# Two-layer network behind attention and experts: depth of the second layer's pipeline, its first and last chunks, and who splits its weights

## The chip, the cores and the metric

The kernel runs on one core of a Trainium2 chip. The metric is the device time of one launch in microseconds (us); lower is better. TensorE is called PE in the profile, VectorE DVE, ScalarE ACT, GpSimd POOL, and SyncE SP.

## The reference

Attention with 4 sink tokens and a window of 128, then a mixture of 8 experts with one expert per token, then a two-layer network. The change touches the last stage alone:

```python
def _moe2_ref(x, w_in, w_out) -> np.ndarray:   # x (3072, 512), w_in (512, 2048), w_out (2048, 512)
    h = x @ w_in
    g = h - np.tanh(h)
    return (g @ w_out).astype(np.float32)
```

## The kernel before, in words

**Stages.** The attention runs to about 205 us of the span and scatters its token rows to their experts' regions. The experts' loop over slots of 128 tokens ends at about 556 us. What follows is the last stage, here called the second layer (functions `up2` and `down2` and their helpers).

**Split numbers.** To keep float32 accuracy, each factor is cut into a high part (a copy rounded to fp32r) and a low part (the difference), and a product is three matmuls: high with high, high with low, low with high. ScalarE makes high parts, VectorE or POOL the low ones. The weights come as quarters of 1 MB into `raw`; a quarter holds two halves of 128x1024. `split_hi` (L747) on ScalarE and `split_lo` (L1356) on POOL or the code at L1252 to L1255 on VectorE split a half. `W_IN` and `W_OUT` are the indices of w_in and w_out behind the 8 experts. `load_raw` on POOL (L1415) fetches the next quarter when both halves of the old one are split.

**Tiling.** 24 tiles of 128 tokens make 6 groups of 4. Per group the hidden width of 2048 is worked in 16 chunks of 128, so there are `STEPS` = 96 chunks in all, numbered n. For a chunk:
- PE: `up2`, 12 matmuls into one of three banks (`HB`), h for 512 tokens.
- ScalarE: `square`, then `tanh` into the one bank `MT`. VectorE: `series` (needs the square). POOL: the last step of the polynomial on `ser`, then the comparison of the square with 1/256 (`s_small`). VectorE: `curve`, three passes: the product (t), the pick of tanh or polynomial by the comparison (`COPY_PREDICATED`), and the subtraction, which gives g_raw and frees the bank. ScalarE: `g_hi`; VectorE: `g_lo`.
- PE: `down2`, for each of the 4 tiles three matmuls that add to the tile's own bank (`YB`) over the 16 chunks. Here it is called the chunk's output product.

**Order around the change.** Each engine's program is written out by hand as a loop over n. PE: `up2(n)`, in chunks 10 to 13 of a group (`TURN`) the turn of one tile of the next group's tokens (`turn_rows`), then `down2(n - 2)`. `up2(n)` waits for g_raw of chunk n - 3, `down2(m)` for g_lo of m. VectorE: `g_lo(n - 2)`, the low part of a turned tile (`tokens_lo`), in chunks 1 to 8 a half of w_out, `series(n)`, `curve(n - 1)`. Behind a group's last output product ScalarE and VectorE copy two tiles each to `raw`, and POOL stores the four by indirect DMA (`store_out`). SP loads the token rows of the next groups into `raw` behind `s_out_lo` or `s_m_turned`.

**Start.** Three tiles of group 0 are turned on PE (tile 0 was already), ScalarE copies their high parts (`tokens_hi`), VectorE makes the low parts, and the first `up2` waits for all three (L713). The gT buffers are a ring of three.

## Time and profile before

| | |
|---|---|
| median of 3 runs | 1114.25 us (1113.52 to 1114.80) |
| the profiled execution | 1115.05 us, its span 1113.3 us |
| busy: PE, DVE, ACT, POOL | 1086.2 us (98%), 606.7 (54%), 482.3 (43%), 492.8 (44%) |
| mean granted clock of TensorE | 0.992 |
| chain that ended last | PE 92%, DVE 3%, POOL 2%, ACT 1%, issue 1%, DMA 1% |
| its largest lines | L705 22%, L697 22%, L630 14%, L644 14% |

The span runs from the first to the last instruction; the execution's own time is 1.75 us longer. The shares of the busy time are means over stages; the windows and the timeline show each stage by itself. The clock is given as a share of full speed: 1 is 2.4 GHz and 0.5 is 1.2 GHz.

### The profile page before, as it was taken

Reading aid. Unit: us, or ns where it says so; the run is one execution under the profiler, and the core shown is the slowest. Engines: PE = TensorE matmul, PEld = TensorE weight load, DVE = VectorE, ACT = ScalarE, POOL = GpSimd, SP = SyncE. Lnnn points to the kernel's source line nnn. Section 1 sums busy time; section 2 is a strip of 40 time slices with the busy share of each in tenths; the row PEclk is TensorE's granted clock in tenths of the full one; section 3 lists DMA queues with packets and bytes.
Section 4 is the critical chain, followed back from the end, with each engine's and each line's share of the span. In section 5 each row is a group of like instructions: output and inputs, shape, how many; then the busy total and the mean of one; then the engine's idle time right before and its main releaser. Section 6 shows DMA issues by size and latency. Waiting matters only on the chain.

```text
span 1113.3 us, 17138 instructions
## 1 busy us (share of the span) xinstructions
PE 1086.2 (98%) x6028; PEld 878.6 (79%) x6028; DVE 606.7 (54%) x1305; ACT 482.3 (43%) x1035; POOL 492.8 (44%) x496
## 2 busy tenths in 40 slices
PE   9999997999999999999989999999999999999995
PEld 6777875888888888888867888888888888888884
DVE  6787785223322232223268666666666666666664
ACT  7898884423241424442444333333333333333332
POOL 3266534707033517481374344335335335335332
PEclk9999999999999999999999999999999999999998
DMA  8636823525124444463232110001011011001000
GB/s 282 203 120 220 255 71 143 189 67 189 47 86 160 124 133 153 136 223 123 96 96 65 29 35 14 20 20 39 10 29 38 1 39 38 1 1 39 1 1 38
DMA packets 37917, 99.44 MB, mean 89 GB/s; under 512 B 8273, under 2 KB 8401, under 8 KB 32721
## 3 DMA queue, kind: packets, MB, share of 16 engines
q1 hardware_dynamic: 29392, 52.30, 15.2%
q0 software_dynamic: 8448, 46.17, 11.9%
q8 instruction: 42, 0.69, 0.3%
q14 instruction: 35, 0.28, 0.1%
HBM read 75.84 MB, written 22.61 MB: 88 GB/s over the span
## 4 chain that ended last, share of the span: by engine, by line
PE 92%; DVE 3%; POOL 2%; ACT 1%; issue 1%; DMA 1%; POOLq 0%; SPq 0%; DVEq 0%; ACTq 0%
PE bank L705 22%; PE bank L697 22%; PE bank L630 14%; PE bank L644 14%; PE bank L446 5%; PE bank L480 4%; PE bank L462 3%; PE bank L636 2%; PE bank L617 1%; PE bank L685 1%; PE bank L524 1%; POOL sq L1452 1%; PE bank L512 1%; PE bank L504 1%; DMA sorted_x<-x_tok,dest 0%
## 5 line engine op out<-in xcount | busy, mean ns | idle before, releaser
L1359 POOL TENSOR_TENSOR weights<-raw,weights 128x1024 fp32r<-128x1024 f32 x72 | 171.3, 2400 | 201.6 <-ACT weights L753 200.5
L697 PE MATMUL bank<-mT_hi,weights 128*128 128x512 f32 x768 | 251.9, 389 | 1.7 <-DVE mT_lo L1184 1.7
L705 PE MATMUL bank<-weights,gT_hi 128*128 128x512 f32 x768 | 241.9, 396 | 6.2 <-DVE gT_lo L1241 6.0
L1451 POOL TENSOR_SCALAR ser<-ser 128x512 f32<-128x512 f32 x96 | 63.9, 665 | 286.5 <-DVE ser L1223 286.3
L705 PEld LDWEIGHTS bank<-weights,gT_hi 128*128 128x128 f32 x768 | 142.1, 189 | 40.6 <-DVE gT_lo L1241 12.2
L697 PEld LDWEIGHTS bank<-mT_hi,weights 128*128 128x128 f32 x768 | 144.2, 188 | 31.8 <-DVE mT_lo L1184 2.0
L705 PE MATMUL bank<-weights,gT_lo 128*128 128x512 f32 x384 | 150.5, 392 | 0.0
L697 PE MATMUL bank<-mT_lo,weights 128*128 128x512 f32 x384 | 149.4, 389 | 0.0
L644 PE MATMUL bank<-weights,hT_hi 128*128 128x512 f32 x464 | 148.6, 401 | 0.0
L918 ACT ACTIVATE bank<-bank 128x512 f32<-128x512 f32 x96 | 55.9, 582 | 213.5 <-DVE ser L1233 213.5
L630 PE MATMUL bank<-weights,mT_hi 128*128 128x512 f32 x464 | 147.5, 399 | 0.0
L1452 POOL TENSOR_SCALAR sq<-sq 128x512 f32<-128x512 f32 x96 | 144.6, 1506 | 0.0
L1188 DVE TENSOR_SCALAR hr<-bank 128x512 f32<-128x512 f32 x29 | 20.1, 692 | 180.3 <-PE bank L630 180.3
L1223 DVE SCALAR_TENSOR_TENSOR ser<-sq 128x512 f32<-128x512 f32 x96 | 67.0, 698 | 83.3 <-ACT sq L910 83.0
L1241 DVE TENSOR_TENSOR gT_lo<-ser,gT_hi 128x512 fp32r<-128x512 f32 x96 | 68.6, 715 | 63.6 <-ACT gT_hi L924 63.6
L761 ACT ACTIVATE prob<-prob,negmax 128x264 f32<-128x264 f32 (+1 forms) x192 | 92.9, 487 | 15.9 <-DVE negmax L975 15.8
L630 PEld LDWEIGHTS bank<-weights,mT_hi 128*128 128x128 f32 x464 | 84.9, 189 | 15.9
L910 ACT ACTIVATE sq<-bank 128x512 f32<-128x512 f32 x96 | 57.3, 597 | 90.2 <-PE bank L697 90.1
L644 PEld LDWEIGHTS bank<-weights,hT_hi 128*128 128x128 f32 x464 | 82.8, 189 | 14.1
L630 PE MATMUL bank<-weights,mT_lo 128*128 128x512 f32 x232 | 91.0, 392 | 0.0
L644 PE MATMUL bank<-weights,hT_lo 128*128 128x512 f32 x232 | 90.8, 391 | 0.0
L705 PEld LDWEIGHTS bank<-weights,gT_lo 128*128 128x128 f32 x384 | 72.4, 189 | 15.7
(154 smaller groups left out, 1584.4 us busy)
## 6 DMA issues: line engine op xcount, KB each, us to landing
raw<-w_all POOLq DMA_DIRECT2D x32, 1024.0 KB, 5.5
raw<-w_all SPq DMA_DIRECT2D x8, 1024.0 KB, 7.6
sorted_y<-ys SPq DMA_DIRECT2D x30, 257.0 KB, 3.3
xs<-sorted_x SPq DMA_DIRECT2D x29, 257.0 KB, 2.8
kT<-kt SPq DMA_DIRECT2D x24, 264.0 KB, 3.1
qT<-qt SPq DMA_DIRECT2D x24, 256.0 KB, 3.9
v_in<-vt SPq DMA_DIRECT2D x24, 256.0 KB, 4.0
raw<-sorted_y SPq DMA_DIRECT2D x20, 257.0 KB, 2.7
```

The lines of the kernel that those rows point to most:

```text
L630: done = e.matmul(bank[MH[n]][:, :], xp[:, c, :], wt[:, c, n * 512:(n + 1) * 512], start=(c == 0 and m == 0), stop=(c == CH - 1 and m == 2))
L644: done = e.matmul(bank[MY][:, :], xp[:, c, :], wt[:, c, :], start=(c == 0 and m == 0), stop=(c == FCH - 1 and m == 2))
L697: done = e.matmul(bank[HB[n % 3]][:, :], wt[:, f // 2, c, cols], x[:, c, :], start=(c == 0 and m == 0), stop=(c == CH - 1 and m == 2))
L705: done = e.matmul(bank[YB[i]][:, :], x[:, n % 3, rows], wt[:, f, :], start=(f == 0 and m == 0), stop=(f == GCH - 1 and m == 2))
L761: e.activation(row, row, ACT.Exp, bias=negmax[:, g % 2, h:h + 1], scale=-1.0, accum_out=rowsum[:, g % 2, h:h + 1]).then_inc(s_exp, 1)
L910: e.activation(sq[:, n % 2, :], bank[HB[n % 3]][:, :], ACT.Square).then_inc(s_sq, 1)
L918: e.activation(bank[MT][:, :], bank[HB[n % 3]][:, :], ACT.Tanh).then_inc(s_tanh, 1)
L1223: e.scalar_tensor_tensor(out=ser[:, n % 2, :], in0=sq[:, n % 2, :], scalar=SERIES_1 / SERIES_2, in1=sq[:, n % 2, :], op0=ALU.add, op1=ALU. ...
L1241: e.tensor_tensor(gT_lo[:, n % 3, :], ser[:, n % 2, :], gT_hi[:, n % 3, :].bitcast(F32), ALU.subtract).then_inc(s_glo, 1)
L1359: e.tensor_tensor(lo, src, hi.bitcast(F32), ALU.subtract).then_inc(s_w_lo, 1)
L1451: e.tensor_scalar(row, row, SERIES_2, 1.0, ALU.mult, ALU.add).then_inc(s_ser, 1)
L1452: e.tensor_scalar(u, u, SMALL_U, None, ALU.is_gt).then_inc(s_small, 1)
```

## The change

- **Depth.** Output products run three chunks behind (`DEPTH`) in place of two. The last two chunks' output products are put tile by tile: both for tile 0, then both for tile 1, and so on.
- **First chunk.** `up2` takes its eight matmuls with high parts of the tokens first and the four with low parts last, in every chunk. The first one waits for the three high parts, of which VectorE copies tile 2's, and before its ninth matmul for the low parts.
- **Comparison.** For chunks 0 and 95 VectorE makes the comparison in place of POOL.
- **Weights.** POOL splits low halves 0 to 4 of w_in and 0 of w_out, all before chunk 0; VectorE halves 5 to 7 of w_in (behind chunks 2, 4, 6) and 1 to 7 of w_out (behind 3, 5, 7 to 11). Before, POOL did all of w_in (the last two at chunks 1 and 2), and VectorE all of w_out. ScalarE's high halves of w_out follow the list `HI_AT`, and POOL's last two loads stand at chunks 3 and 7.
- **VectorE's order.** Up to chunk 11 `g_lo` stands at the end of its own step; in the last two steps the passes of chunks 94 and 95 are interleaved.
- Copies and stores of a group move one step later in each loop; those of the last group stand behind it.

`curve` is cut into `curve_t`, `curve_pick` and `curve_g`, its three passes; `w_in_lo(y)` and `w_out_lo(y)` split half y; `y_copy` is the old copy of a tile under a name.

```diff
-    STEPS, TURN = GROUPS * GCH, 10
+    STEPS, TURN, DEPTH = GROUPS * GCH, 10, 3
+    IN_POOL = 5
...
                     if j == 1:
-                        e.wait_ge(s_out_lo, 2 * i + 2)
+                        if i == 0:
+                            e.wait_ge(s_w_lo, 8 * W_IN + IN_POOL + 1)
+                        e.wait_ge(s_out_lo, 2 * i + 1)
                     else:
...
-                for c in range(CH):
-                    for m, (wt, x) in enumerate(((wih, mT_hi[j % 2]), (wih, mT_lo[j % 2]), (wil, mT_hi[j % 2]))):
-                        done = e.matmul(bank[HB[n % 3]][:, :], wt[:, f // 2, c, cols], x[:, c, :],
-                                        start=(c == 0 and m == 0), stop=(c == CH - 1 and m == 2))
+                high = [(wt, mT_hi[j % 2], c) for c in range(CH) for wt in (wih, wil)]
+                low = [(wih, mT_lo[j % 2], c) for c in range(CH)]
+                for m, (wt, x, c) in enumerate(high + low):
+                    if n == 0 and m == len(high):
+                        e.wait_ge(s_m_lo, GROUP - 1)
+                    done = e.matmul(bank[HB[n % 3]][:, :], wt[:, f // 2, c, cols], x[:, c, :],
+                                    start=(m == 0), stop=(m == 3 * CH - 1))
                 done.then_inc(s_up, 1)
...
-            e.wait_ge(s_m_lo, GROUP - 1)
-            for n in range(STEPS + 2):
+            e.wait_ge(s_m_hi, 2)
+            e.wait_ge(s_m_hi_dve, 1)
+            for n in range(STEPS + DEPTH - 2):
...
                 if n < STEPS:
                     if j == 0 and f % 2 == 0:
-                        e.wait_ge(s_w_lo, 8 * W_IN + f // 2 + 1)
+                        if f // 2 < IN_POOL:
+                            e.wait_ge(s_w_lo, 8 * W_IN + f // 2 + 1)
+                        else:
+                            e.wait_ge(s_in_lo, f // 2 - IN_POOL + 1)
                     if f == 0 and j:
...
+                if n >= DEPTH:
+                    m = n - DEPTH
                     e.wait_ge(s_glo, m + 1)
-                    if m < GCH and m % 2 == 0:
-                        e.wait_ge(s_out_lo, m // 2 + 1)
+                    if m == 0:
+                        e.wait_ge(s_w_lo, 8 * W_IN + IN_POOL + 1)
+                    elif m < GCH and m % 2 == 0:
+                        e.wait_ge(s_out_lo, m // 2)
...
+            e.wait_ge(s_glo, STEPS - 1)
+            for i in range(GROUP):
+                down2(STEPS - 2, i)
+                e.wait_ge(s_glo, STEPS)
+                down2(STEPS - 1, i)
...
+            HI_AT = (1, 3, 5, 7, 8, 9, 10)
...
-            for i, bk in ((1, MT), (2, HB[2]), (3, HB[1])):
+            for i, bk in ((1, MT), (3, HB[1])):
                 tokens_hi(0, i, bk)
             e.wait_ge(s_expert, E)
             split_hi(W_OUT, 0)
...
-                if 1 <= n < 8:
-                    split_hi(W_OUT, n)
+                if n in HI_AT:
+                    split_hi(W_OUT, 1 + HI_AT.index(n))
+                if n < STEPS:
+                    square(n)
+                    tanh(n)
                 if n == 1:
                     e.wait_ge(s_row_ids, GROUP)
                     e.wait_ge(y_all, 1)
-                    g_hi(0)
-                    square(1)
-                    tanh(1)
-                else:
-                    if n < STEPS:
-                        square(n)
-                        tanh(n)
-                    if 2 <= n <= STEPS:
-                        g_hi(n - 1)
...
+                if 1 <= n <= STEPS:
...
+            y_copy(GROUPS - 1, 1, GROUP * (STEPS - 2) + 4)
+            y_copy(GROUPS - 1, 3, GROUP * STEPS)
...
-                e.wait_ge(s_m_hi, GROUP * j + i)
+                if j:
+                    e.wait_ge(s_m_hi, GROUP * j + i - 1)
+                elif i == 2:
+                    e.wait_ge(s_m_hi_dve, 1)
+                else:
+                    e.wait_ge(s_m_hi, (i + 1) // 2)
...
+            def small(n):
+                e.wait_ge(s_w, n + 1)
+                u = sq[:, n % 2, :]
+                e.tensor_scalar(u, u, SMALL_U, None, ALU.is_gt).then_inc(s_small_dve, 1)
...
-                e.wait_ge(s_small, n + 1)
+                if n in (0, STEPS - 1):
+                    e.wait_ge(s_small_dve, 1 if n == 0 else 2)
+                else:
+                    e.wait_ge(s_small, n)
                 e.copy_predicated(row, sq[:, n % 2, :].bitcast(I32), bank[MT][:, :]).then_inc(s_cp, 1)
...
+            e.wait_ge(s_m_turned, 2)
+            e.tensor_copy(mT_hi[0][:, :, 2 * P:3 * P], by_chunk(HB[2])).then_inc(s_m_hi_dve, 1)
             for i, bk in ((1, MT), (2, HB[2]), (3, HB[1])):
                 tokens_lo(0, i, bk)
...
-                if 3 <= n:
+                if 13 <= n < STEPS or n == STEPS + 1:
                     g_lo(n - 2)
...
-                if 1 <= n <= 8:
-                    src, hi, lo = w_half(W_OUT, n - 1)
-                    e.wait_ge(s_w_hi, 8 * W_OUT + n)
-                    e.tensor_tensor(lo, src, hi.bitcast(F32), ALU.subtract).then_inc(s_out_lo, 1)
-                if n == 1:
+                if n == 0:
+                    series(0)
+                    small(0)
+                elif n == 1:
                     curve(0)
+                    series(1)
                     g_lo(0)
-                    series(1)
-                else:
-                    if n < STEPS:
-                        series(n)
-                    if 2 <= n <= STEPS:
-                        curve(n - 1)
-                if n >= 2 and (n - 2) % GCH == GCH - 1:
-                    j2 = (n - 2) // GCH
+                elif n < STEPS - 1:
+                    series(n)
+                    curve(n - 1)
+                    if n in (2, 4, 6):
+                        w_in_lo(IN_POOL + n // 2 - 1)
+                    elif n in (3, 5):
+                        w_out_lo((n - 1) // 2)
+                    elif n <= 11:
+                        w_out_lo(n - 4)
+                    if n <= 11:
+                        g_lo(n - 1)
+                elif n == STEPS - 1:
+                    curve_t(n - 1)
+                    curve_pick(n - 1)
+                    series(n)
+                    curve_g(n - 1)
+                    small(n)
+                elif n == STEPS:
+                    curve_t(n - 1)
+                    g_lo(n - 2)
+                    curve_pick(n - 1)
+                    curve_g(n - 1)
+                if n >= DEPTH and (n - DEPTH) % GCH == GCH - 1:
...
                 nxt = x + 1
-                for j in range(4 if nxt < W_IN else 3):
+                for j in range(4 if nxt < W_IN else 2):
                     split_lo(nxt, 2 * j)
                     split_lo(nxt, 2 * j + 1)
                     e.wait_ge(s_w_lo, 8 * nxt + 2 * j + 2)
                     load_raw(nxt + 1, j)
+            split_lo(W_IN, 4)
+            split_lo(W_OUT, 0)
...
-                    e.tensor_scalar(u, u, SMALL_U, None, ALU.is_gt).then_inc(s_small, 1)
-                if n == 1:
-                    split_lo(W_IN, 6)
-                if n == 2:
-                    split_lo(W_IN, 7)
-                    e.wait_ge(s_w_lo, 8 * W_IN + 8)
+                    if 0 < n < STEPS - 1:
+                        e.tensor_scalar(u, u, SMALL_U, None, ALU.is_gt).then_inc(s_small, 1)
+                if n == 3:
+                    e.wait_ge(s_w_lo, 8 * W_IN + IN_POOL)
+                    e.wait_ge(s_in_lo, 1)
+                    load_raw(W_OUT, 2)
+                if n == 7:
+                    e.wait_ge(s_in_lo, 3)
                     load_raw(W_OUT, 3)
                 if n < STEPS and j + 1 < GROUPS and TURN <= f < TURN + GROUP:
                     e.wait_ge(rows_in[f - TURN], 16 * (j + 1))
                     keep_ids(j + 1, f - TURN)
...
-                if n >= 2 and (n - 2) % GCH == GCH - 1:
+                if n >= DEPTH and (n - DEPTH) % GCH == GCH - 1:
                     for i in range(GROUP):
-                        store_out((n - 2) // GCH, i)
+                        store_out((n - DEPTH) // GCH, i)
+            for i in range(GROUP):
+                store_out(GROUPS - 1, i)
```

The order on PE from the third chunk's end to the fourth's product, before (names: `weights0` holds w_in, `weights1` w_out; banks 1 to 3 are `HB`, 4 to 7 `YB`):

```order
L697 MATMUL bank3<-mT_lo0,weights0 128x512
L697 MATMUL bank3<-mT_hi0,weights0 128x512
L705 MATMUL bank4<-weights1,gT_hi 128x512 [waits w_out_lo,g_lo]
L705 MATMUL bank4<-weights1,gT_hi 128x512
L705 MATMUL bank4<-weights1,gT_lo 128x512
L705 MATMUL bank5<-weights1,gT_hi 128x512 x2
L705 MATMUL bank5<-weights1,gT_lo 128x512
L705 MATMUL bank6<-weights1,gT_hi 128x512 x2
L705 MATMUL bank6<-weights1,gT_lo 128x512
L705 MATMUL bank7<-weights1,gT_hi 128x512 x2
L705 MATMUL bank7<-weights1,gT_lo 128x512
L697 MATMUL bank1<-mT_hi0,weights0 128x512 [waits g_raw]
```

and in the changed kernel, from the first chunk's low parts on:

```order
L707 MATMUL bank1<-mT_lo0,weights0 128x512 [waits m_lo]
L707 MATMUL bank1<-mT_lo0,weights0 128x512 x3
L707 MATMUL bank2<-mT_hi0,weights0 128x512 x8
L707 MATMUL bank2<-mT_lo0,weights0 128x512 x4
L707 MATMUL bank3<-mT_hi0,weights0 128x512 [waits w_lo]
L707 MATMUL bank3<-mT_hi0,weights0 128x512 x7
L707 MATMUL bank3<-mT_lo0,weights0 128x512 x4
L707 MATMUL bank1<-mT_hi0,weights0 128x512 [waits g_raw]
L707 MATMUL bank1<-mT_hi0,weights0 128x512 x7
L707 MATMUL bank1<-mT_lo0,weights0 128x512 x4
L715 MATMUL bank4<-weights1,gT_hi 128x512 [waits w_lo,g_lo]
L715 MATMUL bank4<-weights1,gT_hi 128x512
```

The fourth chunk's product (bank 1, behind `g_raw`) stands ahead of the first output product (bank 4, behind `g_lo`), and the first chunk waits for low parts only at its ninth matmul.

The order on VectorE at the end of the program, before (bank 2 is chunk 94, bank 3 chunk 95, bank 0 `MT`, banks 4 and 6 the output of tiles 0 and 2):

```order
L1223 SCALAR_TENSOR_TENSOR ser<-sq 128x512 [waits g_lo,sq]
L1230 TENSOR_TENSOR ser<-bank2,ser 128x512 [waits tanh,series]
L1233 COPY_PREDICATED ser<-sq,bank0 128x512 [waits small,t]
L1235 TENSOR_TENSOR ser<-bank2,ser 128x512 [waits t_picked]
L1241 TENSOR_TENSOR gT_lo<-ser,gT_hi 128x512 [waits down,g_hi]
L1230 TENSOR_TENSOR ser<-bank3,ser 128x512 [waits tanh,series]
L1233 COPY_PREDICATED ser<-sq,bank0 128x512 [waits small,t]
L1235 TENSOR_TENSOR ser<-bank3,ser 128x512 [waits t_picked]
L1241 TENSOR_TENSOR gT_lo<-ser,gT_hi 128x512 [waits down,g_hi]
L1273 COPY raw<-bank4 128x512 [waits out_done0,down]
L1273 COPY raw<-bank6 128x512 [waits out_done2,down]
```

and in the changed kernel:

```order
L1278 TENSOR_TENSOR ser<-bank2,ser 128x512 [waits tanh,series]
L1287 COPY_PREDICATED ser<-sq,bank0 128x512 [waits small,t]
L1256 SCALAR_TENSOR_TENSOR ser<-sq 128x512 [waits g_lo,sq]
L1292 TENSOR_TENSOR ser<-bank2,ser 128x512 [waits t_picked]
L1262 TENSOR_SCALAR sq<-sq 128x512 [waits series_w]
L1278 TENSOR_TENSOR ser<-bank3,ser 128x512 [waits tanh,series]
L1311 TENSOR_TENSOR gT_lo<-ser,gT_hi 128x512 [waits down,g_hi]
L1287 COPY_PREDICATED ser<-sq,bank0 128x512 [waits small_by_vector,t]
L1292 TENSOR_TENSOR ser<-bank3,ser 128x512 [waits t_picked]
L1311 TENSOR_TENSOR gT_lo<-ser,gT_hi 128x512 [waits down,g_hi]
L1300 COPY raw<-bank4 128x512 [waits down,out_done0]
L1300 COPY raw<-bank6 128x512 [waits down,out_done2]
```

The product and pick of chunk 94 went ahead of chunk 95's series, the comparison of chunk 95 (`TENSOR_SCALAR`) came in, and chunk 95's product stands ahead of chunk 94's low part.

## Rows read from the trace of the kernel before

**Rows 1.** stretches: us, busy (x count) of PE, PEld, DVE, ACT, POOL; clock; DMA share; GB/s
```profile
560.00:600.00 40.00, 36.72 (x151) 29.14 (x152) 29.58 (x36) 17.05 (x26) 26.50 (x23) 0.96 0.28 93
600.00:1089.00 489.00, 488.81 (x2184) 401.49 (x2183) 322.03 (x470) 173.98 (x294) 206.95 (x215) 1.00 0.07 21
```

**Rows 2.** timeline of PE, second layer's start: start us, us, engine line op [idle before <-releaser]
```profile
556.65 1.53 PE L685 MATMUL bank<-ident,rows 128*128 128x128 f32 x12
559.91 0.50 PE L697 MATMUL bank<-mT_hi,weights 128*128 128x512 f32 x1 [1.74 <-DVE mT_lo L1184]
...
567.98 0.39 PE L697 MATMUL bank<-mT_hi,weights 128*128 128x512 f32 x1
570.51 0.90 PE L705 MATMUL bank<-weights,gT_hi 128*128 128x512 f32 x2 [2.14 <-DVE gT_lo L1241]
...
574.94 0.40 PE L697 MATMUL bank<-mT_hi,weights 128*128 128x512 f32 x1
```

**Rows 3.** timeline of ACT, DVE and POOL, from 557 to 569 us
```profile
557.04 4.71 POOL L1359 TENSOR_TENSOR weights<-raw,weights 128x1024 fp32r<-128x1024 f32 x2
...
557.98 1.89 DVE L1184 TENSOR_TENSOR mT_lo<-bank,mT_hi 128x512 fp32r<-128x512 f32 x3 [4.81 <-ACT mT_hi L904]
...
562.97 0.60 ACT L910 ACTIVATE sq<-bank 128x512 f32<-128x512 f32 x1 [3.10 <-PE bank L697]
...
564.21 1.22 DVE L1255 TENSOR_TENSOR weights<-raw,weights 128x1024 fp32r<-128x1024 f32 x1
...
567.51 0.75 DVE L1233 COPY_PREDICATED ser<-sq,bank 128x512 f32<-128x512 int32 x1 [0.88 <-POOL sq L1452]
568.29 0.69 DVE L1235 TENSOR_TENSOR ser<-bank,ser 128x512 f32<-128x512 f32 x1
...
564.38 1.52 POOL L1451 TENSOR_SCALAR ser<-ser 128x512 f32<-128x512 f32 x1 [1.24 <-DVE ser L1223]
```

**Rows 4.** timeline of PE, two later waits of that start
```profile
583.68 0.72 PE L705 MATMUL bank<-weights,gT_hi 128*128 128x512 f32 x2 [0.36 <-DVE gT_lo L1241]
...
590.22 0.73 PE L705 MATMUL bank<-weights,gT_hi 128*128 128x512 f32 x2 [0.79 <-DVE gT_lo L1241]
```

**Rows 5.** timeline of PE, after the last of a group's four turns
```profile
730.53 0.39 PE L697 MATMUL bank<-mT_hi,weights 128*128 128x512 f32 x1
730.96 0.74 PE L705 MATMUL bank<-weights,gT_hi 128*128 128x512 f32 x2
...
752.94 0.74 PE L705 MATMUL bank<-weights,gT_hi 128*128 128x512 f32 x2
```

**Rows 6.** timeline of PE, end of the second layer
```profile
1095.02 0.39 PE L705 MATMUL bank<-weights,gT_lo 128*128 128x512 f32 x1
1097.60 0.73 PE L705 MATMUL bank<-weights,gT_hi 128*128 128x512 f32 x2 [2.19 <-DVE gT_lo L1241]
...
1101.10 0.73 PE L705 MATMUL bank<-weights,gT_hi 128*128 128x512 f32 x2 [0.48 <-DVE gT_lo L1241]
...
1103.75 0.39 PE L705 MATMUL bank<-weights,gT_lo 128*128 128x512 f32 x1
```

**Rows 7.** timeline of DVE and POOL, end of the second layer
```profile
1091.42 0.69 DVE L1241 TENSOR_TENSOR gT_lo<-ser,gT_hi 128x512 fp32r<-128x512 f32 x1 [0.70 <-ACT gT_hi L924]
...
1094.13 0.62 POOL L1451 TENSOR_SCALAR ser<-ser 128x512 f32<-128x512 f32 x1 [3.36 <-DVE ser L1223]
```

**Rows 8.** timeline of DVE, ACT and POOL, the last group's copies and stores
```profile
1102.10 0.69 DVE L1273 COPY raw<-bank 128x512 f32<-128x512 f32 x1 [1.06 <-PE bank L705]
...
1104.17 0.60 ACT L956 ACTIVATE raw<-bank 128x512 f32<-128x512 f32 x1 [0.78 <-PE bank L705]
...
1103.58 1.06 POOL L1439 DMA_INDIRECT out<-raw,ids  x1 [7.37 <-ACT raw L956]
...
1107.48 0.96 POOL L1439 DMA_INDIRECT out<-raw,ids  x1 [0.30 <-issue]
```

**Rows 9.** timeline of DVE, a half of w_out while POOL made a comparison
```profile
583.54 2.51 DVE L1255 TENSOR_TENSOR weights<-raw,weights 128x1024 fp32r<-128x1024 f32 x1
```

57 lines of the change are left out of this document (40 added, 17 removed).

## The prediction

> **What bounds the kernel now.** I read first the stretches of the span, then TensorE's timeline where it is not full, then the engines it waits for. From 600 to 1089 us PE is busy 488.81 of 489.00 us at full clock [rows 1]: nothing there can be gained except by fewer or shorter matmuls, and the change makes neither. From 560 to 600 us it is busy 36.72 of 40 us, with a mean granted clock of 0.96 [rows 1]. So the change can act at four places only: the start of the second layer, tiny lags at each group of tokens, its end, and the tail behind the last matmul. A chunk's product is 12 matmuls; their starts stand 0.23 us apart, and 2.72 us is 12 of them.
>
> The start, in PE's rows [rows 2]: the turns run from 556.65 for 1.53 us, then PE sits idle 1.74 us until VectorE's third low part of the tokens, and begins chunk 0 at 559.91. The third chunk's last matmul starts at 567.98. The first output product starts at 570.51, after 2.14 us idle, waiting for gT_lo of chunk 0; it is not over until 574.94, though 12 matmuls should take 2.72. Its two matmuls at 570.51 take 0.90 us, two plain ones 0.39 + 0.23 = 0.62: the half clock, 1.2 in place of 2.4 GHz. Two more idle pieces follow, of 0.36 and 0.79 us [rows 4].
>
> Why gT_lo of chunk 0 is late [rows 3]: ScalarE squares at 562.97, VectorE's series ends by 564.3, POOL's step on `ser` takes 1.52 us from 564.38, then POOL makes the comparison, and the pick at 567.51 has waited 0.88 us for it; g_raw is there at 568.29 + 0.69 = 568.98; ScalarE's g_hi and VectorE's g_lo follow, and PE goes on at 570.51.
>
> The end [rows 6, 7]: the chain from chunk 95's product to its g_lo is serial, and PE idles 2.19 and 0.48 us before the last two output products. Then [rows 8] tile 3 is copied at 1104.17 to 1104.77, but its store starts at 1107.48: POOL issues the four stores (1107.48 - 1103.58) / 3 = 1.30 us apart, while tiles come 0.68 apart.
>
> **The change part by part.** An idle piece costs PE its idle time and some more: 1095.02 to 1097.60 is 2.58 us, less 0.23 is 2.35, against 2.19 idle (0.16 more), and the first two matmuls behind it take 0.73 in place of 0.62 (0.12 with rounding) [rows 6].
>
> *1. Chunk 0 starts on high parts.* ScalarE copies tiles 1 and 3, VectorE tile 2 beside it, and PE waits for these three alone. The turns end at 556.65 + 1.53 = 558.18; tile 3's copy of 0.60 us (the plain ScalarE copy of a bank [rows 8]) ends at about 558.8, so chunk 0 starts at 558.85. VectorE makes tile 2's copy (0.69, as its other passes over a bank [rows 3]) by 558.4, since the second turn of the three ends at about 557.7, then three low parts, which took 1.89 together [rows 3]: done by 560.3. PE's eight high parts run to 558.85 + 8 x 0.23 = 560.7, so the low parts are in time. **Gain 559.91 - 558.85 = 1.06 us.** That the same 12 matmuls stand in another order costs nothing: each has its own weight load either way.
>
> *2. Three chunks deep.* PE now puts chunk 3's product where the first output product stood. It needs g_raw of chunk 0 alone, which frees bank 1. Everything moves 1.06 earlier: square from 561.91 to 562.51, series to 563.23, POOL's step 0.62 (its plain duration [rows 7]) to 563.93; VectorE makes the comparison itself meanwhile (0.69 or less). Then three passes, 0.69 + 0.75 + 0.69 with 0.02 between [rows 3]: g_raw at 566.15. Chunk 3 is due after 36 matmuls and the first one's 0.11: 558.85 + 8.16 + 0.11 = 567.12. It is early by 1 us. The low half of w_out that VectorE made at 564.21 (1.22 us [rows 3]) is no longer in this chain: POOL makes it ahead. Its two halves of w_in from 557.04 took 4.71 us [rows 3], 2.36 each; now the first is w_in's, to 559.4, the second w_out's, behind ScalarE's high half (ready near 559.9), to 562.3. Then it copies four ids and is free for 563.3. The first output product is due at 569.8 and its g_lo is ready near 567.5. So 567.98 + 0.23 = 568.21 to 574.94, 6.73 us, becomes 2.72. **Gain 4.0 us**, of which 2.3 is the wait and 1.7 the half clock behind it. I take it that the clock stays: what is left of idle is 558.18 to 558.85.
>
> *3. The halves of chunks 2 to 11.* VectorE takes ten halves (three of w_in, seven of w_out) in place of eight, POOL two fewer. They stand behind the three passes of the curve, where VectorE otherwise idled 0.7 us for ScalarE's g_hi. A step of VectorE is then 4 x 0.69 + 0.75 + 1.22 = 4.73 us of work [rows 3] against PE's 5.44 (two products), so it keeps up, and each g_lo has 2.72 us more than before. The two waits at 583.68 and 590.22 go: 0.36 + 0.79 + 2 x (0.16 + 0.12) = 1.71. **Gain 1.7 us.** In chunks 10 and 11 the halves now meet the turns of the next group: from the durations I find the low part of a turned tile ready 2.2 us after the chunk's product ends, due after 0.44 (the turn) + 2.72 = 3.16. POOL's two weight loads move from the expert stage and chunk 2 to chunks 3 and 7, and their high halves are not asked for before chunks 7 and 9, over 10 us later. SP's first row loads wait for the halves of their quarter, the last one for chunk 11's; its tile is turned after chunk 13. Nothing else is queued behind these. Cost 0.
>
> *4. Each later group.* Once per group, after the last turned tile, the output product starts 0.20 late (730.53 to 730.96 is 0.43, not 0.23) and its first matmuls cost 0.12 more; the first product of the next group again 0.12 (0.74 at 752.94) [rows 5]. Both wait for g_lo, and now g_lo has a product's time more. Five groups x 0.44: **gain 2.2 us.** The stores and copies of a group keep their place behind the same product.
>
> *5. The end.* Let T be the end of chunk 95's product: one output product before 1095.02 + 0.23, so 1092.53. Before, three output products follow it, now four, two whole and two by tiles; the total is the same, so only idle time counts. The new order on VectorE, with the passes' durations: g_lo of 93 at T - 1.1 [rows 7]; t and pick of 94 to T + 0.9; series 95 to T + 1.6; g of 94, then the comparison, to T + 2.6 or 2.8; POOL's step on `ser` lies beside them (0.62 [rows 7]). Then t of 95, g_lo of 94, pick and g of 95 to T + 5.4; g_hi (0.6) and g_lo: T + 6.8. PE wants it after 2 products and one tile, T + 6.12. It idles 0.7, with 0.12 behind it 0.8, where it lost 2.19 + 0.48 + 2 x (0.16 + 0.12) = 3.23. **Gain 2.4 us.**
>
> *6. The tail.* The tiles now come 1.36 us apart, slower than POOL's 1.30 per store, so the last store follows its own copy. The first store of the group started at 1103.58, 0.8 us after the first copy's end at 1102.10 + 0.69; with that delay store 3 starts 0.8 behind copy 3, where it was 1107.48 - 1104.77 = 2.71 [rows 8]. **Gain 1.9 us** (2.5 if the delay is 0.2, as from tile 1's copy, which ends 0.6 behind tile 0's).
>
> Sum: 1.06 + 4.0 + 1.7 + 2.2 + 2.4 + 1.9 = 13.3 us. The profiled execution took 1115.05, 0.8 above the median of 1114.25. 1115.05 - 13.3 = 1101.8, and 1101.0 from the median; I take **1101.3 us**.
>
> Two costs no row shows. The comparison on VectorE with operands in SBUF: above, a pass of 0.69; the lower end is 0, and either fits. And whether it disturbs POOL's step on `ser`, which runs beside it. POOL's step took 1.52 at 564.38, beside VectorE's half at 564.21 [rows 3], and 0.62 at 1094.13 [rows 7]: so between 0 and 0.9 at each of the two places. In the start 0.9 eats the 1 us in hand; at the end it puts up to 0.7 on the last g_lo. I take 0, since at the end POOL starts while VectorE is still in its pass on a bank, as in the row of 0.62.
>
> The Trainium skill (SBUF — State Buffer, on the shared port pair) says the two engines lock each other out for whole instructions when VectorE uses both ports or reads two SBUF operands. The 1.52 here and the half of 2.51 us at 583.54 against 1.22 [rows 3, 9] agree: that half ran beside a comparison on POOL. By it the comparison holds POOL off at the start, but there the time in hand covers it.
>
> **Rivals.**
> *A, the clock falls all the same.* PE still stands idle near 558.5, behind turns. For: the only fall in this layer, 0.96 of 40 us being some 3.4 us at half speed, came behind idle time [rows 1, 2]. Against: the larger idle of 1.74 brought none until the second one. Price 1.7: 1103.0. The skill (TensorE: Matmul & The Clock Gate) adds that transposes do not count as busy, which would make 556.65 to 558.85 one empty piece; in this trace 556.65 to 559.91 was longer and the clock held.
> *B, VectorE and POOL in each other's way.* If halves take 2.51 [rows 9], a step of VectorE is 4.73 + 1.29 = 6.0 against 5.44; ten steps lose 5.8, less 2.7 of slack: 3. With 0.7 at the end: 1105.0.
> *C, the wait only changes its place.* If g_raw of chunk 0 comes 2 us or more later than I find, PE idles before chunk 3 and the clock falls as before; 4.0 are not gained: 1105.3.
> *D, slower.* POOL's stores of a group hold it for four times 1.3 us [rows 8], and the next chunk's step on `ser` stands behind them. If the deeper order let that reach PE, before a product that waits for g_raw, each of five groups could stall. It decides only beyond 13.3 / 5 = 2.7 us per group; at 4 us it ends at 1121. Against: stores, copies and product keep their relative order.
> That the change does not do what it says: the order of instructions shows that it does.
>
> **Numbers.** Forecast 0.68 (including its ends of 1099.6 and 1102.3), A 0.11, B 0.09, C 0.08, D 0.02, others 0.02. The range of 8 in 10 goes from 1099.5, with the tail's 2.5 and an end without idle, to 1105.0, taking in A, the bounds and B's own value. Measurement tells 0.2%, 2.2 us, from nothing; all but D lie beyond it: faster 0.96, same 0.02, slower 0.02.
>
> **What would show it.** Chunk 0's product starts about 1.1 us earlier behind the turns; no idle PE before chunk 3; clock 1.00 from 560 to 600; no wait for gT_lo before the last tile pieces, and one of 0.5 to 1 there; the last store some 0.8 behind its copy. A wait at chunk 3, a second wait in the last tiles, or halves of 2 us and more would make it wrong.

## The result and the profile after

The changed kernel takes 1100.39 us (median of 4 runs, 1099.89 to 1101.56), the kernel before 1114.53 us beside it: ratio 0.9874, 95% interval 0.9858 to 0.9889, so 14 us (1.3%) faster. The forecast was 1101.3 us, with a range of 1099.5 to 1105.0. The profiled execution has a span of 1098.7 us.

The stretches of the changed kernel's span, with the columns of [rows 1]:

```profile
560.00:600.00 40.00, 40.00 (x178) 33.12 (x177) 34.30 (x47) 18.83 (x30) 20.92 (x24) 1.00 0.22 79
600.00:1080.00 480.00, 480.00 (x2157) 397.48 (x2156) 321.11 (x468) 173.48 (x293) 207.01 (x213) 1.00 0.07 22
```

From 560 to 600 us PE is full at a clock of 1.00, where it was busy 36.72 us at 0.96 [rows 1]; from 600 to 1080 it is busy without a gap. Its only idle pieces left in the second layer are these two (timeline of PE, start us, us, engine, line, operation, idle before and releaser):

```profile
556.31 1.53 PE L691 MATMUL bank<-ident,rows 128*128 128x128 f32 x12
558.53 2.12 PE L707 MATMUL bank<-mT_hi,weights 128*128 128x512 f32 x8 [0.69 <-ACT mT_hi L926]
560.48 1.07 PE L707 MATMUL bank<-mT_lo,weights 128*128 128x512 f32 x4
...
566.83 1.98 PE L707 MATMUL bank<-mT_hi,weights 128*128 128x512 f32 x8
...
569.55 0.62 PE L715 MATMUL bank<-weights,gT_hi 128*128 128x512 f32 x2
...
1085.51 0.39 PE L715 MATMUL bank<-weights,gT_lo 128*128 128x512 f32 x1
1086.16 0.74 PE L715 MATMUL bank<-weights,gT_hi 128*128 128x512 f32 x2 [0.27 <-DVE gT_lo L1311]
```

They answer to [rows 2] and [rows 6]. Chunk 0 starts 2.22 us after the first turn (before 3.26). Its low parts at 560.48 do not wait. Chunk 3's product begins at 566.83, right behind chunk 2's, and the first output product at 569.55, both without a bracket, so without idle time. At the end 0.27 us are left of 2.19 and 0.48, ahead of the last chunk's product with tile 0.

What releases chunk 3's product, in the timelines of DVE and POOL, against [rows 3]:

```profile
562.22 0.71 DVE L1256 SCALAR_TENSOR_TENSOR ser<-sq 128x512 f32<-128x512 f32 x1 [2.29 <-ACT sq L932]
562.96 0.43 DVE L1262 TENSOR_SCALAR sq<-sq 128x512 f32<-128x512 f32 x1
563.90 0.69 DVE L1278 TENSOR_TENSOR ser<-bank,ser 128x512 f32<-128x512 f32 x1 [0.52 <-POOL ser L1538]
564.63 0.74 DVE L1287 COPY_PREDICATED ser<-sq,bank 128x512 f32<-128x512 int32 x1
565.41 0.69 DVE L1292 TENSOR_TENSOR ser<-bank,ser 128x512 f32<-128x512 f32 x1
...
563.02 0.85 POOL L1538 TENSOR_SCALAR ser<-ser 128x512 f32<-128x512 f32 x1 [0.64 <-DVE ser L1256]
```

VectorE's comparison (L1262) takes 0.43 us and lies beside POOL's step on `ser`, which takes 0.85. The pick at 564.63 waits for nothing, and g_raw is ready at 566.10.

The tail, against [rows 8], timelines of ACT and POOL:

```profile
1091.31 0.60 ACT L948 ACTIVATE raw<-bank 128x512 f32<-128x512 f32 x1 [2.12 <-PE bank L715]
...
1088.70 1.06 POOL L1526 DMA_INDIRECT out<-raw,ids  x1 [6.85 <-DVE raw L1300]
...
1092.81 0.96 POOL L1526 DMA_INDIRECT out<-raw,ids  x1 [0.30 <-issue]
```

The last store starts 0.90 us behind the copy of tile 3 (1091.91); before it was 2.71.

**Where the 14.6 us of span went.** The stretches are measured between the same events in both traces. One output product lasts 2.72 us; the changed kernel carries one more of them from the second stretch to the fourth, and the table corrects for it:

| stretch | before | after | gain | forecast |
|---|---|---|---|---|
| first turn to chunk 0 | 3.26 | 2.22 | 1.04 | 1.06 |
| chunk 0 to the output product behind the first turn of the next group, the carried one added | 58.00 | 49.46 + 2.72 | 5.82 | 5.7 |
| from there to the end of chunk 95's product | 474.62 | 471.62 | 3.00 | 2.2 |
| from there to the last matmul, the carried output product taken off | 11.22 | 11.22 - 2.72 | 2.72 | 2.4 |
| last matmul to the last store | 3.73 | 1.98 | 1.75 | 1.9 |

Together the gains are 14.3 us. Another 0.34 lie ahead of the first turn, where the two programs are alike but for POOL's halves.

### The profile page after: what moved, and what is told of

Same layout as the page of the kernel before. It is cut to its first block, busy times and chain, and to the rows that moved or that the text cites. A ratio compares the mean times of both kernels' runs of the same rounds, so it can differ in the third digit from the quotient of the medians.

```text
span 1098.7 us, 17140 instructions
## 1 busy us (share of the span) xinstructions
PE 1079.1 (98%) x6028; PEld 877.5 (80%) x6028; DVE 609.1 (55%) x1310; ACT 481.7 (44%) x1034; POOL 484.0 (44%) x492
## 4 chain that ended last, share of the span: by engine, by line
PE 95%; DVE 1%; DMA 1%; issue 1%; ACT 1%; SPq 0%; POOL 0%; POOLq 0%; ACTq 0%; DVEq 0%
PE bank L707 24%; PE bank L715 23%; PE bank L636 15%; PE bank L650 15%; PE bank L452 5%; PE bank L486 4%; PE bank L468 3%; PE bank L642 2%; PE bank L623 1%; PE bank L691 1%; PE bank L530 1%; PE bank L518 1%; PE bank L510 1%; DMA qT<-qt 0%; DMA sorted_x<-x_tok,dest 0%
## 5 line engine op out<-in xcount | busy, mean ns | idle before, releaser
L1444 POOL TENSOR_TENSOR weights<-raw,weights 128x1024 fp32r<-128x1024 f32 x70 | 166.6, 2401 | 201.7 <-ACT weights L775 200.6
L715 PE MATMUL bank<-weights,gT_hi 128*128 128x512 f32 x768 | 238.6, 392 | 0.3 <-DVE gT_lo L1311 0.3
L707 PE MATMUL bank<-mT_hi,weights 128*128 128x512 f32 x768 | 189.8, 389 | 0.7 <-ACT mT_hi L926 0.7
L1540 POOL TENSOR_SCALAR sq<-sq 128x512 f32<-128x512 f32 x94 | 140.6, 1496 | 0.0
L707 PE MATMUL bank<-mT_lo,weights 128*128 128x512 f32 x384 | 102.7, 389 | 0.0
L650 PEld LDWEIGHTS bank<-weights,hT_hi 128*128 128x128 f32 x464 | 82.9, 189 | 14.1
```

Of the source, the lines that this page charges most:

```text
L650: done = e.matmul(bank[MY][:, :], xp[:, c, :], wt[:, c, :], start=(c == 0 and m == 0), stop=(c == FCH - 1 and m == 2))
L707: done = e.matmul(bank[HB[n % 3]][:, :], wt[:, f // 2, c, cols], x[:, c, :], start=(m == 0), stop=(m == 3 * CH - 1))
L715: done = e.matmul(bank[YB[i]][:, :], x[:, n % 3, rows], wt[:, f, :], start=(f == 0 and m == 0), stop=(f == GCH - 1 and m == 2))
L1444: e.tensor_tensor(lo, src, hi.bitcast(F32), ALU.subtract).then_inc(s_w_lo, 1)
L1540: e.tensor_scalar(u, u, SMALL_U, None, ALU.is_gt).then_inc(s_small, 1)
```

## The experiments

The part of the program ahead of the second layer ends at another time in each execution (the first turn starts between 554.9 and 558.9 us, and the clock falls once, twice or not at all in the attention). So beside the timing I compare one length within the profile: **L, from the start of chunk 0's product to the start of the last matmul**. It is 543.84 us before, 532.30 after, and 532.28 in the changed kernel's second profile (e12), so in these two it repeats to 0.02 us. L leaves out the wait ahead of chunk 0 and the stores at the end. Each value of L comes from one profiled execution.

### The end by tiles undone (e1)

```diff
             e.wait_ge(s_glo, STEPS - 1)
-            for i in range(GROUP):
-                down2(STEPS - 2, i)
-                e.wait_ge(s_glo, STEPS)
-                down2(STEPS - 1, i)
+            for n in (STEPS - 2, STEPS - 1):
+                e.wait_ge(s_glo, n + 1)
+                for i in range(GROUP):
+                    down2(n, i)
...
```

The waits of the last four copies are fitted to this order.

> The changed kernel with the last two output products whole again (chunk 94 for all four tiles, then chunk 95), nothing else. My theory: PE loses its last idle piece (0.27 us in the changed kernel's trace, 0.55 with what lies around it), since three whole products last 8.2 us and chunk 95's low part is there after 6.5; but the tiles come 0.68 us apart again, POOL's stores 1.3, so the last store starts 2.7 us behind the copy of tile 3 instead of 0.9. Sum 1.8 - 0.55 = 1.3 us slower, about 1101.6. Rival: the order by tiles is there against PE's wait and the stores do not matter; then it is as fast or 0.5 us faster, and the last store starts 0.9 us behind its copy.

Measured: 1099.92 us, ratio 0.9878 (0.9862 to 0.9895). L is 531.76, 0.54 shorter, and PE has no idle piece at the end. The stores (timelines of ACT and POOL):

```profile
1089.68 0.60 ACT L947 ACTIVATE raw<-bank 128x512 f32<-128x512 f32 x1 [0.76 <-PE bank L715]
...
1089.12 1.06 POOL L1525 DMA_INDIRECT out<-raw,ids  x1 [8.35 <-ACT raw L947]
...
1093.01 0.96 POOL L1525 DMA_INDIRECT out<-raw,ids  x1 [0.30 <-issue]
```

The last store starts 2.73 us behind the last copy (1090.28). So both halves of the theory hold in the profile: 1.83 us are lost at the stores and 0.54 won on PE, 1.3 us in sum. The timing cannot tell 1.3 us from nothing: its interval holds the changed kernel's ratio. In the profile the order by tiles pays through the stores, not through PE's wait.

### Depth two (e2) and depth alone (e8)

e2 is the changed kernel with

```diff
-    STEPS, TURN, DEPTH = GROUPS * GCH, 10, 3
+    STEPS, TURN, DEPTH = GROUPS * GCH, 10, 2
```

and the loops of copies and stores bounded to fit; e8 is the kernel before, its 2 replaced by such a `DEPTH` of 3 in PE's loop and in the copies and stores, and nothing else.

> The changed kernel with depth 2 instead of 3, all else kept (first chunk, split of the halves, VectorE's order, order by tiles at the end). My theory: PE idles about 1.2 us before the first output product (its low part was ready at 567.94, chunk 2's product ends at 566.7), 0.3 around it; the lags once or twice per group return, 2.5 us; at the end 2.7 us return. Sum 7.0 us, 1107.4, with the clock at 1.00 from 560 to 600 us; if an idle piece of 1.2 us is enough to bring the clock down, 1.7 more, 1109.1. Rival: the moved halves and VectorE's order made the gain and depth little: then within 2 us of the changed kernel.

> The kernel before with depth 3 alone: no high parts first, no halves moved, VectorE's and ScalarE's orders as before, last products whole. My theory: depth is the largest part. Chunk 3's product waits for g_raw of chunk 0, 568.98 against 568.21, so PE idles 0.6 us (0.3 more around it) where it lost 4.0; the two later waits (1.7) and the lags of the groups (2.4) go; at the end about 0.3 us idle are left of 3.2 lost. Gain 3.1 + 1.7 + 2.4 + 2.6 = 9.8 us, about 1104.3. Rival: without the new order VectorE and POOL stay late in the first chunks, PE waits for g_raw instead of g_lo at several of chunks 3 to 8, and the gain is 6 us or less, 1108.

Measured, e2: 1109.60 us, ratio 0.9961 (0.9947 to 0.9975), L 542.20, so 9.9 us of 11.5 are gone. PE's waits in its timeline:

```profile
567.42 0.73 PE L715 MATMUL bank<-weights,gT_hi 128*128 128x512 f32 x2 [0.98 <-DVE gT_lo L1311]
...
618.82 0.73 PE L715 MATMUL bank<-weights,gT_hi 128*128 128x512 f32 x2 [0.76 <-DVE gT_lo L1311]
...
1091.11 0.74 PE L715 MATMUL bank<-weights,gT_hi 128*128 128x512 f32 x2 [0.89 <-DVE gT_lo L1311]
...
1093.87 0.73 PE L715 MATMUL bank<-weights,gT_hi 128*128 128x512 f32 x2 [1.80 <-DVE gT_lo L1311]
```

The first wait is 0.98, near the 1.2 expected, and the clock holds behind it. I had not expected the 0.76 us behind the second turn (chunk 11), where a half of w_out stands ahead of g_lo on VectorE, nor the fall of the clock at 1094.9 for 3.4 us, behind the two idle pieces at the end. They make most of the difference between 9.9 and 7.0.

Measured, e8: 1110.57 us, ratio 0.9938 (0.9921 to 0.9954), on a chip where the kernel before takes 1117.97. L is 537.31: 6.5 us won, not 9.8. **The rival's mechanism is the one that came**, with a gain a little above its 6. PE now waits for g_raw, four times in the first chunks:

```profile
570.59 0.50 PE L697 MATMUL bank<-mT_hi,weights 128*128 128x512 f32 x1 [0.65 <-DVE ser L1235]
...
577.82 0.47 PE L697 MATMUL bank<-mT_hi,weights 128*128 128x512 f32 x1 [1.49 <-DVE ser L1235]
...
583.79 0.50 PE L697 MATMUL bank<-mT_hi,weights 128*128 128x512 f32 x1 [0.25 <-DVE ser L1235]
...
590.40 0.47 PE L697 MATMUL bank<-mT_hi,weights 128*128 128x512 f32 x1 [0.86 <-DVE ser L1235]
```

and once more, 0.40 us, at the first turn of the next group. The chain of that stretch (what each piece of work waited for, followed back from the end) runs from ScalarE's g_hi of chunk 0 over VectorE's g_lo of chunk 0 and its series of chunk 1 to POOL, and stays on POOL until its load at 584.61 (start us, us, what):

```profile
570.65 0.64 ACT gT_hi L924
...
571.32 0.69 DVE gT_lo L1241
572.01 0.61 DVE ser L1223
...
572.69 1.53 POOL ser L1451
574.22 1.89 POOL sq L1452
576.11 2.33 POOL weights L1359
578.44 1.09 POOL ser L1451
579.53 2.42 POOL sq L1452
581.96 2.37 POOL weights L1359
```

The step on `ser` takes 1.53 and 1.09 us for 0.62, the comparison 1.89 and 2.42 for 1.49, and between them stand w_in's halves of 2.33 and 2.37. So depth alone brings 6.5 of 11.5 us of L, all the rest without it 1.6, and 3.4 come only when both are there. By the stretches of the table in the section on the result, with gains against the kernel before:

| stretch | changed kernel | depth two (e2) | depth alone (e8) |
|---|---|---|---|
| chunk 0 to the output product behind the first turn | 5.82 | 4.08 | 0.80 |
| from there to the end of chunk 95's product | 3.00 | -0.83 | 2.98 |
| from there to the last matmul | 2.72 | -1.61 | 2.75 |

The gains at the groups and at the end come with depth alone in full. At the start it is the other way round: most of the gain is there without the third chunk of depth, and depth alone brings little.

The first of e8's four waits can be accounted for. g_raw of chunk 0 is ready 9.05 us after chunk 0's start, in the changed kernel 7.57. The comparison on POOL makes 0.59 of the difference (e4, below), and POOL's step, 1.52 us beside VectorE's half of w_out in place of the 0.62 of e4, makes the other 0.90.

### Which of the rest (e9, e10)

e9: POOL makes halves 6 and 7 of w_in at chunks 1 and 2 again. e10: VectorE's old order in chunks 2 to 11.

```diff
...
-                    if n in (2, 4, 6):
-                        w_in_lo(IN_POOL + n // 2 - 1)
+                    if n == 2:
+                        w_in_lo(IN_POOL)
+                    elif n in (4, 6):
+                        pass
...
+                if n in (1, 2):
+                    split_lo(W_IN, 5 + n)
...
```

```diff
-                if 13 <= n < STEPS or n == STEPS + 1:
+                if 3 <= n < STEPS or n == STEPS + 1:
                     g_lo(n - 2)
...
-                    series(n)
-                    curve(n - 1)
                     if n in (2, 4, 6):
                         w_in_lo(IN_POOL + n // 2 - 1)
                     elif n in (3, 5):
                         w_out_lo((n - 1) // 2)
                     elif n <= 11:
                         w_out_lo(n - 4)
-                    if n <= 11:
-                        g_lo(n - 1)
+                    series(n)
+                    curve(n - 1)
```

> The changed kernel, but POOL splits halves 6 and 7 of w_in again, at chunks 1 and 2, as in the kernel before; all else kept. It asks what made depth alone (e8) wait for g_raw. Theory P: POOL's two halves, 2.4 us each, stand ahead of its step on ser for chunks 2 and 3 and make g_raw late; then PE waits before chunks 4 to 6, some 2 us or more in sum. Theory V: it is VectorE's half standing ahead of series, beside POOL's work. By the durations in the changed kernel's trace, POOL's step of chunk 2 would come at 571.7 and of chunk 3 at 576.2, both before VectorE asks for them at 573.8 and 578.4: then PE does not wait, 0 to 0.3 us slower.

> The changed kernel, but in chunks 2 to 11 VectorE's order is the old one: g_lo of two chunks back first, then the half of the weights, then series, then the curve. POOL has no halves there. Theory V: the half delays series, POOL's step and comparison run beside the next half, both are drawn out (2.5 us instead of 1.22 for a half), and PE waits before several chunks for g_raw: 2 us or more slower. Theory P: POOL's halves were the cause in e8; then here PE has no wait in chunks 3 to 12, 0 to 0.3 us slower.

Measured, e9: 1099.21 us, ratio 0.9871 (0.9855 to 0.9888), L 532.35: nothing is lost, though the two engines do stretch each other (timelines of POOL and DVE):

```profile
567.86 2.40 POOL L1446 TENSOR_TENSOR weights<-raw,weights 128x1024 fp32r<-128x1024 f32 x1
570.23 1.59 POOL L1540 TENSOR_SCALAR ser<-ser 128x512 f32<-128x512 f32 x1
571.79 1.93 POOL L1542 TENSOR_SCALAR sq<-sq 128x512 f32<-128x512 f32 x1
...
569.56 1.78 DVE L1267 TENSOR_TENSOR weights<-raw,weights 128x1024 fp32r<-128x1024 f32 x1
571.27 1.10 DVE L1311 TENSOR_TENSOR gT_lo<-ser,gT_hi 128x512 fp32r<-128x512 f32 x1
```

POOL's step is 1.59, VectorE's half 1.78.

Measured, e10: 1100.57 us, ratio 0.9883 (0.9867 to 0.99), L 533.51, 1.2 longer, all in one wait at the first turn:

```profile
609.33 0.66 PE L691 MATMUL bank<-ident,raw 128*128 128x128 f32 x4 [0.94 <-DVE ser L1292]
```

So neither P nor V, put back by itself, brings e8's waits. In the changed kernel each delay fits into what is in hand: POOL's halves wholly, VectorE's order except at the first turn.

Beside the new chunk 0, both runs keep one thing that e8 lacks, and no run tests it alone: the order at chunk 1. In e8, as in the kernel before, ScalarE makes g_hi of chunk 0 ahead of chunk 1's square, and VectorE g_lo of chunk 0 ahead of chunk 1's series. So chunk 1's square starts 9.70 us after chunk 0's start in e8 (571.19) and 5.78 after it in the changed kernel (564.31). POOL's step for chunk 1 starts 11.20 us after it in e8, and 8.25, 8.25 and 8.24 in the changed kernel, e9 and e10. POOL's and VectorE's halves thus meet 3 us more in hand in e9 and e10 than in e8; 1.48 of them are chunk 0's earlier g_raw, the rest goes with that order. Which combination of this order, the halves, and POOL's comparison and the half at chunk 0 makes e8's later waits was not tried and stays open.

### The start: waiting for the low parts (e3)

```diff
+                if n == 0:
+                    e.wait_ge(s_m_lo, GROUP - 1)
                 for m, (wt, x, c) in enumerate(high + low):
-                    if n == 0 and m == len(high):
-                        e.wait_ge(s_m_lo, GROUP - 1)
```

> The changed kernel, but chunk 0 waits for the three low parts before its first matmul; the order of the matmuls and VectorE's copy of tile 2 stay. My theory: chunk 0 starts when the third low part ends, 559.93 in the changed kernel's trace, so at 559.97 instead of 558.53: 1.4 us slower, 1101.8, and nothing else moves, since everything behind shifts with it. Rival: the longer idle piece behind the turns brings the clock down soon after: 1.7 more, 1103.5.

Measured: 1101.59 us, ratio 0.9898 (0.9882 to 0.9915). Chunk 0 starts 3.76 us after the first turn, 1.54 later; L is unchanged at 532.28. Timeline of PE, and the stretch behind it:

```profile
559.78 2.06 PE L706 MATMUL bank<-mT_hi,weights 128*128 128x512 f32 x8 [2.23 <-DVE mT_lo L1211]
560.00:600.00 40.00, 40.00 (x178) 33.10 (x178) 33.19 (x45) 18.58 (x29) 19.37 (x23) 1.00 0.19 65
```

The idle piece of 2.23 us behind the turns brings no fall. Expected was a start 1.4 us later and no fall.

### The comparison back on POOL (e4)

In the edit, `small(0)` and `small(95)` leave VectorE and POOL makes all 96 comparisons.

> The changed kernel with the comparisons of chunks 0 and 95 on POOL again. My theory: the comparison on VectorE is worth almost nothing, since three chunks of depth leave g_raw of chunk 0 early enough: POOL's step (0.62 alone) and comparison (1.49) end at about 565.1, the pick starts 0.5 us later, g_raw is ready at 566.6 and due at 566.75. At the end POOL's comparison would be ready at 1083.3, where the pick started at 1083.25. So 0 to 0.2 us slower, 1100.5. Rival: POOL's comparison is drawn out beside VectorE (1.93 us at 567.37) or counts in full: PE idles 0.4 us or more before chunk 3, and at the end 0.5 more: 1101.3 or above.

Measured: 1100.24 us, ratio 0.988 (0.9863 to 0.9896), L 532.59, 0.29 longer. Timelines of DVE and POOL:

```profile
566.28 0.74 DVE L1284 COPY_PREDICATED ser<-sq,bank 128x512 f32<-128x512 int32 x1 [0.88 <-POOL sq L1535]
567.05 0.69 DVE L1289 TENSOR_TENSOR ser<-bank,ser 128x512 f32<-128x512 f32 x1
...
564.06 0.62 POOL L1533 TENSOR_SCALAR ser<-ser 128x512 f32<-128x512 f32 x1 [0.64 <-DVE ser L1256]
564.66 1.52 POOL L1535 TENSOR_SCALAR sq<-sq 128x512 f32<-128x512 f32 x1
```

The pick waits 0.88 us for POOL as before the change, g_raw comes 0.59 later against chunk 0's start (8.16 for 7.57), and PE still does not wait before chunk 3; at the end its idle piece is 0.44 instead of 0.27. So the comparison on VectorE is worth 0.3 us of L, too little for the timing. POOL's step takes 0.62 here, 0.85 with the comparison on VectorE beside it: that 0.23 is the cost that I had bounded by 0 and 0.9 and taken as 0.

### What an idle piece costs (e5, e6, e7)

One more wait ahead of chunk 3's product in the changed kernel, on `s_glo, 1`, on `s_w, 3` and on `s_graw, 2`:

```diff
                     if n >= 3:
                         e.wait_ge(s_graw, n - 2)
+                    if n == 3:
+                        e.wait_ge(s_glo, 1)
```

> The changed kernel with one added wait: chunk 3's product also waits for the low part of chunk 0 (there at 567.94; chunk 2's product ends at 566.7). It prices a short idle piece of PE. My theory: PE idles 1.2 us, 0.3 more around it, the clock stays at 1.00 behind it: 1.5 us slower, 1101.9. Rival: the idle piece is enough for a fall of the clock: 1.7 more, 1103.6.

> The changed kernel with one added wait: chunk 3's product also waits for VectorE's series of chunk 2 (there at 568.95). PE idles 2.2 us, as long as before the first output product of the old kernel. My theory, by the old kernel's trace, where 2.14 us idle were followed by a fall: the clock falls to half for 3.4 us, 2.2 + 0.3 + 1.7 = 4.2 us slower, 1104.6. Rival: it was the two idle pieces within 10 us of each other, 1.74 and 2.14, that brought it down, and here with 0.69 and 2.2 it stays: 2.5 us slower, 1102.9.

> The changed kernel with one added wait: chunk 3's product also waits for g_raw of chunk 1 (there at 571.06). PE idles 4.3 us. My theory: the clock falls for 3.4 us, once: 4.3 + 0.3 + 1.7 = 6.3 us slower, 1106.7. Rival: the fall lies within the idle piece itself and costs nothing beyond it, 4.6 us slower, 1105.0.

Measured: 1104.06, 1107.03 and 1109.96 us, ratios 0.988 (0.9863 to 0.9896), 0.9905 (0.9888 to 0.9922) and 0.9927 (0.991 to 0.9944), on the chip of e8. L is 533.66, 536.28 and 539.59. Timelines of PE, for e6 with one window behind the wait, for e7 with three, one across the wait's end and two behind it (columns as in [rows 1]; the clock is the third number from the end):

```profile
570.29 0.93 PE L707 MATMUL bank<-mT_hi,weights 128*128 128x512 f32 x3 [1.08 <-DVE gT_lo L1313]
```

```profile
571.72 3.05 PE L707 MATMUL bank<-mT_hi,weights 128*128 128x512 f32 x8 [2.11 <-DVE ser L1258]
572.00:576.00 4.00, 4.00 (x12) 3.10 (x11) 3.35 (x5) 2.16 (x3) 1.97 (x2) 0.57 0.00 0
```

```profile
573.68 3.75 PE L707 MATMUL bank<-mT_hi,weights 128*128 128x512 f32 x8 [4.19 <-DVE ser L1294]
572.00:576.00 4.00, 2.32 (x6) 1.89 (x7) 3.20 (x5) 2.16 (x3) 1.83 (x2) 0.62 0.00 0
576.00:580.00 4.00, 4.00 (x11) 3.16 (x10) 0.19 (x1) 0.60 (x1) 0.00 (x0) 0.52 0.00 0
580.00:600.00 20.00, 20.00 (x90) 16.53 (x89) 16.63 (x23) 7.63 (x13) 8.86 (x9) 1.00 0.18 66
```

With 1.08 us idle nothing follows: L grows by 1.36. With 2.11 us the eight high parts take 3.05 us instead of 1.98: the clock is at half for 3.4 us from 572.6 on, and L grows by 3.98, of which 1.7 is the clock. With 4.19 us it grows by 7.29, 1.0 more than my theory and 2.7 more than the rival: the clock is at half for 6.8 us from 573.0 on, of which 0.7 lies within the idle piece, and half of the other 6.1 comes on top of the 4.19. So the step "the clock stays" was worth the 1.7 it was put at, and could have been worth more. Each of these lengths is of one execution. The medians agree in kind: the ratios lie 0.0005, 0.0030 and 0.0052 above e12's 0.9875, which is 0.6, 3.4 and 5.8 us, each ratio uncertain by 1.9 us.

The Trainium skill (TensorE: Matmul & The Clock Gate, "What's actually happening") ties the fall to idle time and the return to activity. The runs agree in kind: 1.08 us of idle time brought no fall, 2.11 and 4.19 did. The Trainium skill also says (same page, "PE-mode transpose") that a transpose does not count as busy in the same way. By that, e3 had 3.76 us of transposes and idle time, and even its idle piece alone, 2.23 us, was longer than e6's 2.11; e3 brought no fall and e6 did. So the length of the idle piece alone does not decide it, and what does no run here shows.

### The last chunk in halves (e11), and the changed kernel again (e12)

```diff
-                e.wait_ge(s_glo, STEPS)
+                e.wait_ge(s_glo, STEPS + i // 2)
                 down2(STEPS - 1, i)
...
+            def g_lo_half(n, half):
+                at = slice(2 * P * half, 2 * P * half + 2 * P)
+                e.wait_ge(s_ghi, n + 1 + half)
+                e.wait_ge(s_down, GROUP * (n - 2))
+                e.tensor_tensor(gT_lo[:, n % 3, at], ser[:, n % 2, at], gT_hi[:, n % 3, at].bitcast(F32),
+                                ALU.subtract).then_inc(s_glo, 1)
```

with the subtraction to g_raw and `g_hi` of chunk 95 cut in the same way.

> A version that may beat both: the changed kernel with the last three passes of chunk 95 (g_raw, g_hi, g_lo) each in two halves of 256 columns, so that tiles 0 and 1 need only the first halves. From the durations of passes over 512 columns (0.69, 0.63, 0.69 one after the other) the first halves should be there some 0.7 us earlier, PE's last idle piece of 0.27 goes with the 0.28 around it, and the end comes 0.5 us earlier; too little for the timing, so the profile decides. Rival: a pass of half the columns costs nearly as much as a whole one, the second halves are late and PE idles before tile 2.

> The changed kernel once more, as the base line of this call on this chip: 14 us faster than the kernel before, ratio 0.987 to 0.988.

Measured: e11 1098.65 us, ratio 0.9865 (0.9849 to 0.9882); e12 1099.15 us, ratio 0.9875 (0.9859 to 0.9892). L is 531.73 in e11, 0.55 shorter than in e12, and PE is idle nowhere behind chunk 0's start. VectorE's last passes:

```profile
1083.26 0.73 DVE L1296 COPY_PREDICATED ser<-sq,bank 128x512 f32<-128x512 int32 x1
1084.02 0.76 DVE L1319 TENSOR_TENSOR ser<-bank,ser 128x256 f32<-128x256 f32 x2
1084.93 0.76 DVE L1326 TENSOR_TENSOR gT_lo<-ser,gT_hi 128x256 fp32r<-128x256 f32 x2 [0.15 <-ACT gT_hi L957]
```

Two half passes take 0.76 us together, one whole 0.69, but the first low half is there in time. The 0.55 us are shown by the profile; the timing does not resolve them. e12 gives the changed kernel's ratio again, 0.9875 beside 0.9874.

## Why the prediction was right

The forecast of 13.3 us stands against 14.1 by the medians. The waits went where it said, step by step; what it did not tell apart is how little of steps 2 and 3 the depth itself brings.

- *Step 1*, 1.06 us: 1.04. In e3, where PE waits for the low parts again, chunk 0 comes 3.76 us after the turns and not the 3.26 of before, because VectorE now copies tile 2 ahead of its low parts, which end 3.61 us after the turns' start instead of 3.22 (559.63 less 556.02, and 559.87 less 556.65): by these times the copy moved to VectorE pays only together with the high parts first.
- *Steps 2 and 3*, 4.0 and 1.7: 5.82 together. g_raw of chunk 0 was forecast for 566.15 and came at 566.10, but that is luck: chunk 0 itself began 0.32 us earlier than forecast. Counted from its start, g_raw came after 7.57 us where 7.30 was forecast, since POOL's step took 0.85 and not 0.62, and chunk 3's product began after 8.30 where it was due after 8.27; the time in hand was 0.7 us, not 1. The clock stayed, as taken; e6 shows that an idle piece like the old one of 2.14 us brings it down again. The prediction put the 4.0 us under "Three chunks deep". Depth is the smaller part of it: without it 4.08 of the 5.82 us are there (e2), because g_lo of chunk 0 already comes early enough to leave PE idle 0.98 us in place of 2.14, with no fall of the clock behind it. Depth alone brings 0.80 (e8), since new waits for g_raw stand in place of the old ones. Rival C named this mechanism, but only for chunk 0, and it needed the old schedule to be kept. The statement that each of the ten halves costs 1.22 us held for all ten, from 570.97 to 618.13; e9 shows stretched ones.
- *Step 4*, 2.2: 3.0. This term was too small. I had read 0.44 us in each group, a lag of 0.20 and twice 0.12. The two late products also run slowly to their ends (730.96 to 733.85 and 752.94 to 755.83 are 2.89 us each, not 2.72), and the second starts 0.04 late: 0.58 a group, 2.9 in five. e8 shows the whole gain with depth alone.
- *Step 5*, 2.4: 2.72. The comparison on VectorE took 0.47 and not 0.69, and the last low part was ready 6.5 us behind T (the end of chunk 95's product), not 6.8.
- *Step 6*, 1.9: 1.75, for a delay of 0.90 from copy to store instead of 0.8. e1 shows the other side: with tiles 0.68 us apart the delay is 2.73.
- Rivals A (the clock falls all the same), B (halves at 2.51 us) and D (stores that stall a group) did not happen: the clock stays at 1.00, the halves take 1.22, and no group shows a wait.

## What to carry to other kernels

This pipeline, which one engine bounds, lost time only where it fills, drains, or turns; read those stretches by themselves, and add the clock to the price of an idle piece there. Moving the consumer one stage back pays only as far as the producer's next wait is not as late: before taking the whole gain, put the new wait (here g_raw in place of g_lo) against its own due time, chunk by chunk. When a change has several parts, give each stretch its own split: here depth made the gains at the groups and at the end, and the earlier results of VectorE and POOL most of the gain at the start. At the drain, compare the spacing of the results with what the next stage needs for each; work put in order of results can cost the bound engine something and still end earlier.
